# Transposes and logits of the normalized rows moved into the attention loop, and a softmax over tokens in two groups

## The reference

```python
# attention with the 32 largest scores of each row
scores = scale * q @ k^T                      # 4 batches, 8 heads, 576 tokens, head size 64
kth = 32nd largest of each row;  scores[scores < kth] = -1e9
attn = softmax(scores);  x = (attn @ v)       # then x: 2304 tokens x 512

# soft mixture: 8 experts, 4 slots each
logits = x @ phi                              # 2304 x 32
d = softmax of logits over the 2304 tokens;   slot_input = d^T @ x      # 32 x 512
slot_out = relu(slot_input @ w1[e]) @ w2[e]
c = softmax of logits over the 32 slots;      x = c @ slot_out

# top-2 mixture: noisy gate picks two of 8 experts for each token
out = sum over the two of  gate * relu(x @ w1[e]) @ w2[e]
```

## Time and profile before

| | us |
|---|---|
| median of 3 runs (lowest, highest) | 1070.72 (1069.97, 1071.25) |
| the profiled execution | 1072.71 |
| its span, first to last instruction | 1070.9 |
| TensorE, VectorE busy | 962.8, 785.2 |
| ScalarE, GpSimd busy | 612.2, 621.4 |
| end of the loop, start of the experts' first products | 626.2, 674.0 |

### The profile page before, as it was taken

The page is one execution under the profiler, slowest core; times in us unless marked ns, Lnnn a source line. Parts: engine busy times, 40 slices in busy tenths (PEclk is TensorE's granted clock), DMA queues, the critical chain, the costliest instruction groups (busy, mean ns, idle before and its releaser), DMA issues.

```text
span 1070.9 us, 21707 instructions
## 1 busy us (share of the span) xinstructions
PE 962.8 (90%) x6439; PEld 674.3 (63%) x6439; DVE 785.2 (73%) x1511; ACT 612.2 (57%) x1243; POOL 621.4 (58%) x940
## 2 busy tenths in 40 slices
PE   3899998999999999999999989997699999999995
PEld 1566666666666666666666676332377878777884
DVE  5999999999999999999999963105735443554251
ACT  2787887787778878778878872102323332333121
POOL 3577777777777777777777760001444544555453
PEclk9999999999999999999999999998899999999998
DMA  9910110110110010010010006899915534433332
GB/s 349 421 46 34 47 30 15 45 45 12 33 45 12 33 45 12 33 45 21 24 45 12 0 1 229 329 420 422 384 22 120 120 42 113 117 42 41 43 41 32
DMA packets 23776, 105.14 MB, mean 98 GB/s; under 512 B 3200, under 2 KB 4288, under 8 KB 16576
## 3 DMA queue, kind: packets, MB, share of 16 engines
q1 hardware_dynamic: 15856, 84.54, 20.6%
q0 software_dynamic: 7168, 11.21, 8.0%
q10 hardware_dynamic: 720, 8.98, 2.3%
HBM read 88.39 MB, written 16.07 MB: 98 GB/s over the span
## 4 chain that ended last, share of the span: by engine, by line
PE 31%; DVE 28%; issue 23%; POOL 6%; DMA 6%; ACT 3%; DVEq 1%; SPq 1%; POOLq 0%; ACTq 0%
PE psum L843 14%; DVE arena L1049 8%; PE psum L848 7%; DVE arena L1045 6%; DVE arena L1037 5%; DVE arena L1033 3%; POOL arena L1334 3%; DMA arena<-w_top 2%; ACT h_hi L1009 2%; DVE arena L1053 2%; DMA arena<-xs_rows,arena 2%; POOL arena L1371 2%; DVE arena L1041 2%; PE psum L830 1%; PE psum L719 1%
## 5 line engine op out<-in xcount | busy, mean ns | idle before, releaser
L1334 POOL TENSOR_SCALAR arena<-arena 128x576 bf16<-128x576 f32 x144 | 249.5, 1733 | 135.5 <-DVE arena L1033 128.5
L586 PE MATMUL psum<-arena 128*128 128x130 f32 (+3 forms) x1600 | 220.6, 279 | 2.8 <-ACT arena L891 2.8
L586 PEld LDWEIGHTS psum<-arena 128*128 128x128 f32 (+3 forms) x1600 | 185.6, 178 | 35.7 <-ACT arena L891 3.3
L543 PE MATMUL psum<-arena 64*128 64x288 f32 (+1 forms) x640 | 111.8, 462 | 58.1 <-DVE arena L1041 53.1
L1293 DVE COPY arena<-psum 128x512 f32 x41 | 28.3, 691 | 152.9 <-PE psum L848 120.5
L843 PE MATMUL psum<-w_hi,h_hi 128*128 128x512 f32 x320 | 131.4, 411 | 6.5 <-ACT h_hi L1009 1.8
L871 ACT ACTIVATE arena<-arena 128x576 bf16<-128x576 bf16 x144 | 98.6, 685 | 64.6 <-POOL arena L1334 64.5
L1009 ACT ACTIVATE h_hi<-psum 128x512 fp32r<-128x512 f32 x80 | 43.4, 595 | 160.3 <-PE psum L830 159.5
L843 PE MATMUL psum<-w_lo,h_hi 128*128 128x512 f32 x320 | 126.9, 396 | 0.0
L1037 DVE MAX8 arena<-psum 128x8 f32<-128x576 f32 x144 | 109.3, 759 | 14.4 <-PE psum L555 13.3
L865 ACT COPY arena<-psum 128x576 f32<-128x576 f32 x144 | 90.6, 629 | 38.4 <-PE psum L543 38.1
(11 more groups left out here) (198 smaller groups left out, 1629.2 us busy)
## 6 DMA issues: line engine op xcount, KB each, us to landing
weights<-w_soft SPq DMA_DIRECT2D x21, 1024.0 KB, 16.1
arena<-qkv SPq DMA_DIRECT2D x15, 864.0 KB, 4.4
weights<-w_top SPq DMA_DIRECT2D x12, 1024.0 KB, 25.9
arena<-w_soft SPq DMA_DIRECT2D x11, 1024.0 KB, 9.5
weights<-w_top SPq DMA_DIRECT2D x3, 2048.0 KB, 26.6
weights<-w_top ACTq DMA_DIRECT2D x3, 2048.0 KB, 7.9
arena<-qkv SPq DMA_DIRECT2D x16, 325.0 KB, 2.9
out<-arena SPq DMA_DIRECT2D x1, 4864.0 KB, 18.3
```

What stands on the lines that cost most here:

```text
L543: last = nc.tensor.matmul(bank(2 * (t % 2) + x, SH)[q0:q0 + rows, :], qT[u][half, w * P + q0:w * P + q0 + rows], kT[u][half, h * SH:(h + 1 ...
L586: last = nc.tensor.matmul(o_place(n, k)[0:rows, :], wT[0:kr, t % 2, kc, q0:q0 + rows], v_, start=(kc == 0), stop=(kc == KC - 1))
L1334: nc.gpsimd.tensor_scalar(hit[t % 2], s_sb[t % S_SLOTS], m8[t % S_SLOTS][:, 7:8], None, ALU.is_ge) \
```

## The change

The loop is restructured into two written iterations (0 and 1) and three rounds of a loop body of two. From iteration 1 on, in every iteration, x of the iteration before is transposed in steps 2, 6 and 7 through bank 7 and its logits are formed in steps 3, 7 and 8 in bank 6, partitions 64 to 127; ScalarE copies the transposes to `xT_main` and `xT_rem`, and the logits of finished batches to `logits_T`. GpSimd normalizes into one of two fixed places of `x16`, and SyncE copies from there to the place of the iteration. `keep_warm` is left out in steps 2, 3, 6, 7 and 8.

```diff
-            steps(pe, [(0, qk_a), (1, strike_b), (LAG_T, trans), (LAG_O, keep_warm), (0, qk_b), (0, strike_a),
-                       (LAG_O, attn_v)], lambda m: a_work(early_tiles(m)))
+            steps(pe, [(0, qk_a), (1, strike_b), (LAG_T, trans), (LAG_O, keep_warm), (None, x_work), (0, qk_b),
+                       (0, strike_a), (None, x_taken), (LAG_O, attn_v)])
...
+        X_STEPS = (2, 6, 7)
+            def x_work(now, half, n):
+                if isinstance(now, int) and now == 0:
+                    return
+                j, odd = now - 1, 1 - half
+                if n == 3 or n == 7:
+                    u = n // 7
...
+                    hold(pe, xt_c, 3 * j + u + 1)
+                    logits(2 * odd + u, 0, D).then_inc(lg, 1)
+                if n in X_STEPS:
+                    pe.wait_ge(o_copied, DPI * now + n - LAG_O + 1)
+                    if n == 2:
+                        hold(pe, x_done, DPI * j + 8)
+                        x_trans(odd, 0, 7)
+                    else:
+                        hold(pe, x_done, DPI * j + 12)
+                        (x_trans(odd, 1, 7) if n == 6 else rest_trans(odd, 7))
+                if n == 8:
+                    hold(pe, xt_c, 3 * j + 3)
+                    rest_logits(j, odd)
+            def x_taken(now, half, n):
+                if n in X_STEPS and not (isinstance(now, int) and now == 0):
+                    hold(pe, xt_c, 3 * (now - 1) + X_STEPS.index(n) + 1)
...
             steps(act, [(0, copy_a), (1, count_b), (LAG_T, wt_a), (LAG_T, wt_b), (0, count_a), (0, copy_b),
-                        (LAG_K, exp_a), (LAG_K, exp_b), (LAG_K, below_a), (LAG_K, below_b), (LAG_O, copy_o)],
-                  lambda m: xT_even(early_tiles(m)))
+                        (None, x_copy_t), (LAG_K, exp_a), (LAG_K, exp_b), (LAG_K, below_a), (LAG_K, below_b),
+                        (LAG_O, copy_o)])
...
+            def x_copy_t(now, half, n):
...
+                if n in X_STEPS:
+                    i = X_STEPS.index(n)
+                    hold(act, xt, 3 * j + i + 1)
...
+                    (nc.scalar.copy(xT_main, bank(7)) if i < 2 else nc.scalar.copy(xT_rem, bank(7, 2 * REM))) \
+                        .then_inc(xt_c, 1)
...
+        def keep_x(eng, j, odd):
+            hold(eng, x_done, DPI * j + 12)
+            eng.dma_start(x16[:, j, :, :], x16[:, KEPT + odd, :, :]).then_inc(x_kept, 16)
+            eng.dma_start(rest_j[0:REM, j, :], rest_j[0:REM, KEPT + odd, :]).then_inc(x_kept, 16)
+            with sp.Fori(2, KEPT, 2) as j:
+                load_pairs(j)
+                keep_x(sp, j - 1, 1)
+                load_pairs(j + 1)
+                keep_x(sp, j, 0)
```

```diff
+            strike_b(LAST, DPI - 1)
+            trans(LAST, DPI - 3)
+            pe.wait_ge(x_done, DPI * LAST + 8)
+            pe.wait_ge(struck16, TPI * ITERS + 1)
+            x_trans(1, 0, 0)
+            attn_v(LAST, DPI - 3)
+            trans(LAST, DPI - 2)
+            pe.wait_ge(xt_c, 3 * LAST + 1)
+            logits(2, 0, D).then_inc(lg, 1)
+            pe.wait_ge(wt_copied, DUOS)
+            pe.wait_ge(e7_set, 1)
...
+            pe.wait_ge(o_copied, DUOS - 1)
+            av_last(DPI - 2, 7, wT, 0)
+            pe.wait_ge(wt8_act, 2)
+            pe.wait_ge(wt8_dve, 1)
+            av_last(DPI - 1, 1, wT_last, 0)
+            pe.wait_ge(soft_exp, 1)
...
+            pe.wait_ge(x_near, 2)
+            nc.tensor.transpose(bank(2, P), x16[:, LAST, NC - 1, P:2 * P], ident).then_inc(xt, 1)
+            rest_trans(1, 7)
...
+            logits(3, 3 * P, D).then_inc(lg, 1)
...
+            pe.wait_ge(t_act, 1)
+            for m in range((B - 1) * NC):
...
+            last.then_inc(soft_sum, 1)
...
+            pe.wait_ge(soft_exp, 2)
...
+            for c in range(NC):
+                nc.tensor.matmul(by_pair(bank(5)[32 * c:32 * c + 32, :]), late_w[:, c * SL:(c + 1) * SL],
+                                 x_rows((B - 1) * NC + c), start=True, stop=False, skip_group_check=True)
...
-            pe.wait_ge(st, 6)
+            pe.wait_ge(slot_set, 2)
+            pe.wait_ge(slot_act, 1)
```

More of the change, by code:

```diff
@@ new lines, in logits, with rest_logits @@
+            def logits(k, first, last_):
+                return nc.tensor.matmul(bank(6, last_ - first, first)[slots_of, :], phi_sb[:, k, :],
+                                        xT_main[:, first:last_], start=(k == 0), stop=(k == DC - 1),
+                                        skip_group_check=True)
+            def rest_logits(j, odd):
+                if not isinstance(j, int) and odd == 0:
+                    hold(pe, rest_kept, j)
+                for u in range(2):
+                    k = 2 * odd + u
+                    last = nc.tensor.matmul(bank(6, REM)[rests_of, :], phi_sb[:, k, :], xT_rem[:, u * REM:(u + 1) * REM],
+                                            start=(k == 0), stop=(k == DC - 1), skip_group_check=True)
+                last.then_inc(lg, 1)
@@ new lines, in _ @@
+            pe.wait_ge(x_near, 1)
+            pe.wait_ge(struck16, TPI * ITERS + 2)
+            for c in range(NC - 1):
+                last = nc.tensor.transpose(bank(3, P, c * P), x16[:, LAST, c, P:2 * P], ident)
+            last.then_inc(xt, 1)
+            pe.wait_ge(x_near, 2)
+            nc.tensor.transpose(bank(2, P), x16[:, LAST, NC - 1, P:2 * P], ident).then_inc(xt, 1)
+            rest_trans(1, 7)
+            pe.wait_ge(xt_c, 3 * LAST + 2)
+            logits(3, 0, 3 * P)
+            pe.wait_ge(xT_dve, 1)
@@ new lines, in _ @@
+            pe.wait_ge(small_in, 48)
+            pe.wait_ge(soft_stat, 3)
+            nc.tensor.matmul(bank(0, 2, 15 * SL), more[slots_of, M_SAME:M_SAME + P], stat[slots_of, 12:14],
+                             start=True, stop=True).then_inc(soft_ps, 1)
+            pe.wait_ge(t_dve, 1)
+            for c in range(NC):
+                nc.tensor.matmul(by_pair(bank(5)[32 * c:32 * c + 32, :]), late_w[:, c * SL:(c + 1) * SL],
+                                 x_rows((B - 1) * NC + c), start=True, stop=False, skip_group_check=True)
@@ new lines, in _ @@
+            pe.wait_ge(t_act, 2)
+            for b in range(B):
+                last = nc.tensor.matmul(bank(5)[32 * b:32 * b + 32, :], late_w[0:REM, (NC + b) * SL:(NC + b + 1) * SL],
+                                        rest[0:REM, b, :], start=False, stop=True, skip_group_check=True)
+            last.then_inc(soft_sum, 1)
+            for m in range(8, TT):
+                last = raw(m)
+            last.then_inc(raw_ps, 1)
+            pe.wait_ge(slot_set, 1)
+            for k in range(DC):
+                last = nc.tensor.matmul(bank((7, 0)[k // 2], P, (k % 2) * P), part[:, k * P:(k + 1) * P],
+                                        more[:, M_PERM:M_PERM + P], start=True, stop=True)
+                if k % 2:
+                    last.then_inc(soft_ps, 1)
```

579 lines of the change are left out of this document (343 added, 236 removed).

## The result

| | before | after |
|---|---|---|
| median of the runs, us (lowest, highest) | 1070.89 (1069.97, 1071.25) | 1107.16 (1102.3, 1108.65) |
| the profiled execution, its span | 1072.71, 1070.9 | 1102.3, 1100.5 |
| 0 to the last strike of the loop | 626.3 | 667.6 |
| last strike to the experts' first product | 47.7 | 31.0 |
| first product to the end | 396.9 | 401.9 |

The change makes the kernel 3.4% slower: ratio 1.0339, 95% interval 1.0306 to 1.0373. The forecast was 1076.5 us with a range of 1055 to 1090, so the direction was right and the time lies 17 us above the range. Of the three stretches the drain came out as forecast. The loop grew by 41.4 us where 22.5 were forecast, and the stretch behind the drain by 5.0 where nothing was. The profiled execution is the fastest of the four; the others lie 4.6 to 6.4 us above it, at a lower mean clock (0.957 to 0.961, against 0.967).

What follows compares the result with a forecast made beforehand. VectorE, 98.6% busy, bounds the loop in a closed ring of waits with TensorE. From the profiled 1072.7 us, +24.5 - 2.0 - 16.6 = +5.9 gives 1078.6, as a median 1076.5 us; range 1055 to 1090.

Steps and rivals of the forecast that it cites:

- x_taken: Loop steps 2, 6 and 7: TensorE's attn_v waits for ScalarE's copy of the transposes; +24.5 us, bounds 18 and 31.
- new work in the loop: Loop: transposes and logits products take the fillers' place and TensorE's idle time, so their own work adds nothing.
- clock in the loop: TensorE's clock in the loop: the sum assumed it stays at full rate and counted nothing for it.
- drain and softmax: Last strike to the experts' first product: 31.1 us in place of 47.7, -16.6 us, bounds -13 and -19.
- behind it: From the experts' first product to the end: everything moves rigidly with that product, stretch as long as now, 396.9 us.
- third rival: Loop: attn_v behind the waits runs at 1.2 GHz, 3 us more each, up to +63 us; chance 0.06.
- first rival: Loop: attn_v does not wait for the copy, or VectorE is not delayed; 1052 us, chance 0.22 for 1048 to 1066.
- Back edges: Loop turns: six back edges and an entry become two and an entry, saving four times 0.48; -2 us, bounds 0 and -3.
- SyncE: Loop: two SBUF-to-SBUF copies an iteration, ahead of the next pair's q and k load, cost nothing.
- The signs foretold: If right: iterations of 80.5 instead of 77.4 us, VectorE about 94% busy; if the clock falls: below 1.00 in loop windows.

Runs made afterwards that it cites:

- wait filled: Changed kernel with six unread 512-column products on TensorE ahead of the wait before attn_v: 1083.41 us against 1070.51, ratio 1.0111.
- copy moved: Changed kernel with ScalarE's copies of the transposes moved ahead of its count: 1056.57 us against 1070.51, ratio 0.9877.
- body of two: Kernel before with only iteration 1 written out and a loop body of two iterations: 1068.3 us against 1071.19, ratio 0.998.

## Why the prediction was wrong in size

| term | forecast | measured | by which runs |
|---|---|---|---|
| `x_taken`, delay at full clock | +24.5 | +26.2 | wait filled 565.18, copy moved 538.95 |
| iteration 1 written out, body of two | -2.0 | -4.6 | body of two 537.39, before 541.98 |
| new work in the loop | 0 | +1.6 | copy moved 538.95, body of two 537.39 |
| clock in the loop | 0 | +18.1 | after 583.25, wait filled 565.18 |
| drain and softmax | -16.6 | -16.7 | the two profiles |
| behind it | 0 | +5.0 | the two profiles |
| sum | +5.9 | +29.6 | spans: 1100.5 less 1070.9 = 29.6 |

The four rows of the loop are the seven iterations of one profile each, between like instructions.

The other runs of the changed kernel are 4.6 to 7.8 us above the profiled one. Their mean clock is lower, but they have no profile, so that the clock makes that difference is likely and not shown.

*The step that failed* is the weighing of the clock: the third rival, given 0.06, is what happened on top of the forecast. It was refused on "91% busy in the drain with no fall" and single idle times of 0.95 us. The drain before has three of these, and no wait of 1.4 us in a loop that comes back to it. The experiments take share and waits apart: 87% busy with idle times up to 1.14 us, but no wait ahead of `attn_v`, keeps the clock; waits of 1.1 us and more ahead of `attn_v` lose it in part of the cases with all fillers in place; and the changed kernel's waits, filled, keep it. The sum put the clock at nothing, and it measured +18.1 us. The rival's price was 3 us a wait and +21 for a third of them, which is close to what came: eight falls of 21 waits, 2.3 us each (of the 18.1, 47.0 less 29.4, 17.6, stand in VectorE's idle time). It is less than 3 because the clock came back a few microseconds on and `attn_v` spent only part of its time at the lower level. Why just these waits lose the clock stays open. The prediction named the Trainium skill, "TensorE: Matmul & The Clock Gate", section "A second HAM failure mode: psum-queue depth-cycling": small idle times between groups of products can make the clock swing between its levels. The trace of the changed kernel agrees (eight falls behind 21 waits), that of the kernel before without fillers does not (35 idle times of 1.04 to 1.14 us and no fall). The forecast should have given it more than 0.06. By the rule no size follows; that had to come from the runs.

*x_taken.* Place and cause were right, and the price nearly. In the written-out iteration the distance from copy to `attn_v` is about the 0.06 us assumed. In the body it is 0.34 us more, which stood only in the upper bound, and yet the sum of the delays is 26.2 and not 31: the rest of the working was some 0.2 us too high at each wait (in iteration 1 the first wait is 1.26 us, not 1.43). It came out near in part by two errors that cancel.

*The first rival*, the copy not waited for, was priced at 1052 us; the kernel with the copy moved is that case, and took 1056.6, of which 3.0 lie behind the drain (399.9 against 396.9).

*Back edges*: iterations 2 to 7 of the restructured old kernel save the forecast 2 us; the 2.5 us of the written-out iteration 1 were not forecast. *SyncE*, GpSimd's new waits, transposes and logits: together at most the 1.6 us of the table. *The drain*: 31.0 against 31.1, with `attn_v`, the 50 short products (5.9 against 5.5) and the combining steps near their forecasts. But it holds only at full clock. The changed kernel and the first one with the copy moved have it; the five other profiles with the new drain take 32.6 to 36.3 us, and in every one of them the granted clock of the drain is below 1.00 (0.81 to 0.95). The forecast's bounds for the drain had no such term.

*Behind it* "moves rigidly" held in kind and not in size. Where GpSimd's indirect transfers meet VectorE's long instructions and ScalarE's load is a matter of a microsecond, and it came out differently with the new drain. The count of slow scatters parts the profiles: none or one in the seven whose stretch is 394.5 to 397.8 us, two to seven in the six at 399.7 to 404.1. The kernel with the new drain at 395.8 has one, as has the old drain with the body of two. That they cause the difference is not shown: two go with +5.0 us, seven with +2.8. Why the kernels with the new drain mostly come out 3 to 7 us longer stays open; the one load that was tried is not it.

*The signs foretold.* An iteration was to take 80.5 us: between like waits of VectorE it takes 80.9 with the wait filled (352.89 to 433.81) and 83.9 in the changed kernel with one fall in it (358.25 to 442.19). VectorE was to be 94% busy, and is with the wait filled (526.75 of 556.2, 94.7%), 91.7% in the changed kernel. "A clock below 1.00 in the windows of the loop" was written down as the sign of the third rival, and it was there: 0.97.

## What to carry to other kernels

A wait put on an engine that runs in order is priced by what stands behind it, and on TensorE there is a second price, the clock. The length of the longest idle time that a kernel has survived is no safe measure: 35 idle times of up to 1.14 us lost nothing here, and waits of 1.11 us at another place did, in some executions. Before adding such a wait, look for idle time on the engine that releases it: ScalarE had 0.68 us right ahead of an instruction in the same step, and moving one entry of its list turned 3.4% slower into 1.1 to 1.2% faster. Where the wait can't go, unread products in it kept the clock of the loop, and cost nothing that the wait had not already cost.

## What was not expected of the hardware

- Waits of 1.1 to 1.8 us on TensorE, three in some 80 us, brought the clock to 1.2 GHz in part of the cases, and the times differ between executions of one kernel (1095.7 and 1110.7 us; 1092.9 and 1102.5 us), with the mean clock. 35 idle times of 1.04 to 1.14 us, five in 77 us, did not.
- Unread products left out cost 1.8 us where there are no waits and 16.5 where there are.
- Two register-valued waits that are already fulfilled cost TensorE 0.33 to 0.34 us when they stand behind the wait that blocks, and nothing seen when they stand ahead of it.
- GpSimd's issue of an indirect scatter took 2.97 to 3.68 us instead of 1.60 in each of the 28 cases in which it began within 0.81 us of the start of VectorE's two subtractions of 128x2048, and ended 3.77 or 3.78 us after that start.
